# q and k fetched one head further ahead, W1 in eight smaller pieces, and the hash bits of both column halves in one bank

## The chip, the core and the metric

The kernel runs on one core of one Trainium2 chip. The time is that of the device, in microseconds, for one launch. Most executions of one kernel agree closely, but three runs of this one spread over 13 us (below). A tensor product is made by TensorE (PE), element work by VectorE (DVE), ScalarE (ACT) and GpSimd (POOL); transfers are issued from the queues of SyncE (SP) and POOL and are carried by the same 16 DMA engines.

## What is computed

```python
def _attn_ref(q, k, v, proj):                      # 2 x 8 heads, 768 rows, head_dim 64
    scale = 1.0 / np.sqrt(D)
    q_bits = (np.einsum('bhsd,dk->bhsk', q, proj) > 0)      # 6 bits per row
    k_bits = (np.einsum('bhsd,dk->bhsk', k, proj) > 0)
    mask = q_bucket[:, :, :, None] == k_bucket[:, :, None, :]
    scores = scale * np.matmul(q, k.transpose(0, 1, 3, 2))
    scores = np.where(mask, scores, -1000000000.0)
    attn = softmax(scores)
    return np.matmul(attn, v)

x = attention output as (2, 768, 512)
x = u + relu(norm(u) @ w_ch1) @ w_ch2,  u = x + real(fft2(x))
out = u2 + relu(u2 @ w_ch),  u2 = x + w_tok_r @ (x cos(x w_theta)) + w_tok_i @ (x sin(x w_theta))
```

All of it is float32. The kernel gets that precision by splitting each operand into a high part and the rest, and multiplying three times.

## The kernel before

The program runs through four stages: attention over 16 heads (to about 270 us of the span), the two Fourier products and the norm (to about 345 us), the network with W1 and W2, and the token mixing. The change touches attention and the transfer of W1 that runs beside it.

**The slots.** `schedule()` lays attention out in slots. A slot is one tile of 128 query rows; a head has six, t = 0 to 5. In a slot PE makes the tile's scores (four products, lines 771 and 772), then the six transposes (746) of the tile two slots back in two units "eta" and "etb", then four products with v (786, 787) for the tile five slots back, which add up in one bank `OT`, and last the slot's extra units. There are two kinds of these: "bits" of the next head in slots 0 and 1 (three products each, lines 724 to 726, one column half each), and "back" in slots 3 and 5 (three transposes, line 757). The units share three PSUM banks in turn (`ring`), and a unit waits until the one three before it has been copied out.

**What follows on the other engines.** For each tile DVE takes the row maxima of the scores (`negmax`, 993), makes from them the factor and bias of the exponential (`affine`, 996, a 128x2 operation whose inputs both lie in SBUF), and subtracts the high part of the transposed tile (`ETL`, 1003, twice). ACT copies out the transposed tile (`ETH`, 619), then takes the exponential (`E`, 626), which needs `affine`, and in slots 1 and 4 it then copies out the finished bank of the v products (`OS`, 635). PE can start the next v products, in slots 2 and 5, only when that copy is done. DVE also makes `einv` (1022, 1024) once a head, in slot 3.

**The mask.** The bits of q and k of the next head enter its scores as 12 further rows of the second product (`QM`, `KM`). ACT copies the bits from PSUM to `MB` (643), one half in slot 0 and one in slot 1. POOL turns them into rows (`mask_rows`, 507: `MR`, 24x768), and SP moves these rows under q and k with two transfers (426, 427). The first head's rows are made by DVE (1017).

**POOL, per head, in order:** `finish` (516, 519) of the head before, `mask_rows` for head h + 1, `scale_q` (492) for head h + 2, the split of q and k of head h + 2 into high and low part (`split_top`: 500 and 502, the latter with two inputs in SBUF), `finish`, `split_v` (535, 537). POOL takes these as soon as what they wait for is there; nothing ties them to a slot. In slots 2 and 5 it also issues one of the waiting transfers in `early`: twelve tables, then W1 in four transfers of 1 MB, so that two go out per head.

**SP, per head, in order:** `move_away(h)` (410, 411), `load_qk(h + 1)` (392), `move_in(h)` (417, 418), `move_mask(h)` (426, 427), `load_v(h + 1)` (397). It waits in order: a transfer that waits holds all behind it. `QK` has two buffers, filled by turns.

## Time and profile before

| what | value |
|---|---|
| runs, us | 796.34, 809.35, 806.29 |
| median, us | 806.29 |
| the profiled execution, us | 805.94 |
| its span, us | 803.8 |
| mean granted clock of PE, share of full speed | 0.968 |
| busy share of the span: PE, DVE, ACT, POOL | 93%, 55%, 40%, 36% |
| POOL mask rows (L507), 15 of them, mean ns | 2933 |
| idle of POOL before them, waiting for ACT's copy of the bits, us | 43.6 |
| idle of PE before the scores, waiting for the mask transfer (3 times), us | 9.1 |
| idle of PE before the v products, waiting for ACT's OS (13 times), us | 4.0 |

The profile is of one execution; its times are counted from the start of its span. A row of the trace gives the start, the duration, the engine, the line and what is written from what; a bracket at its end says how long the engine had been idle and what released it. Matmuls overlap in the records, so PE's pace is read from the distance between starts.

### The profile page before, as it was taken

The page shows a single profiled execution, that of the slowest core. Times are in us where ns is not written, and L with a number is a line of the kernel's source. Part 1 is how long each engine was busy: PE and PEld are TensorE (multiplying, and loading weights), DVE is VectorE, ACT ScalarE, POOL GpSimd, SP SyncE. Part 2 cuts the span into 40 slices and gives each one's busy share as a digit, 9 for nine tenths or more (in the row PEclk, how much of TensorE's full clock was granted, in tenths as well). Part 3 has the DMA queues.
Part 4 walks back from the last instruction along what each step waited for, and adds up shares of the span by engine and source line. Part 5 has one row for each costly group of instructions (what it writes and reads, how often), then busy time and mean ns, then how long its engine had stood idle before and what let it go on. Part 6 is the DMA issues. An engine that isn't in the chain of part 4 may idle for free.

```text
span 803.8 us, 10972 instructions
## 1 busy us (share of the span) xinstructions
PE 745.3 (93%) x3826; PEld 625.6 (78%) x3826; DVE 445.5 (55%) x770; ACT 318.3 (40%) x659; POOL 286.9 (36%) x275
## 2 busy tenths in 40 slices
PE   4999989989999769799999999999995998999998
PEld 2788888878898557688888888888874787888876
DVE  2998997889998688522212122211127565855433
ACT  2889887879899211211111111011014342322201
POOL 3788977668772376335000000200002114312100
PEclk9999999999999869799999999999998999999999
DMA  5366548733430134712000001300002231000002
GB/s 146 94 154 170 136 93 203 192 89 87 113 73 5 53 114 135 210 40 78 1 1 1 0 1 47 99 0 1 1 31 81 60 92 40 1 14 21 19 27 78
DMA packets 44679, 56.25 MB, mean 70 GB/s; under 512 B 15956, under 2 KB 27860, under 8 KB 44116
## 3 DMA queue, kind: packets, MB, share of 16 engines
q1 hardware_dynamic: 38100, 41.65, 19.3%
q0 software_dynamic: 6528, 13.92, 6.1%
q8 instruction: 32, 0.52, 0.3%
q14 instruction: 19, 0.16, 0.1%
HBM read 38.65 MB, written 3.15 MB: 52 GB/s over the span
## 4 chain that ended last, share of the span: by engine, by line
PE 75%; DVE 14%; issue 4%; DMA 3%; ACT 2%; POOL 1%; SPq 1%; ACTq 0%; POOLq 0%
PE PS L724 20%; PE PS L726 19%; PE PS L725 19%; DVE negmax L993 4%; PE PS L746 3%; DVE ETL L1003 3%; PE PS L786 3%; PE PS L771 2%; PE PS L772 2%; PE PS L787 2%; DVE affine L996 2%; DMA KM<-MR 2%; PE PS L907 1%; PE PS L914 1%; PE PS L757 1%
## 5 line engine op out<-in xcount | busy, mean ns | idle before, releaser
L1113 DVE SCALAR_TENSOR_TENSOR HL<-PS,HH 128x512 fp32r<-128x512 f32 x48 | 33.2, 692 | 188.6 <-ACT HH L687 188.6
L687 ACT ACTIVATE HH<-PS 128x512 fp32r<-128x512 f32 x48 | 28.7, 598 | 210.4 <-PE PS L726 210.4
L626 ACT ACTIVATE E<-PS,affine 128x768 f32<-128x768 f32 x96 | 95.3, 992 | 35.7 <-DVE affine L996 33.0
L993 DVE TENSOR_REDUCE negmax<-PS 128x1 f32<-128x768 f32 x96 | 90.9, 947 | 28.4 <-PE PS L772 27.5
L1003 DVE TENSOR_TENSOR ETL<-PS,ETH 128x384 fp32r<-128x384 f32 x192 | 97.1, 545 | 1.2 <-ACT ETH L619 1.2
L619 ACT ACTIVATE ETH<-PS 128x384 fp32r<-128x384 f32 x192 | 83.4, 488 | 9.6 <-PE PS L746 9.0
L746 PE MATMUL PS<-ident,E 128*128 128x128 f32 x576 | 82.1, 276 | 4.2 <-DVE ETL L1003 4.2
L771 PE MATMUL PS<-TOPH,TOPL 128*128 128x512 f32 x192 | 69.8, 364 | 9.4 <-DMA KM<-MR 9.1
L724 PE MATMUL PS<-UTH,W1H 128*128 128x512 f32 x192 | 76.8, 400 | 1.7 <-DVE UTL L1096 1.7
L786 PE MATMUL PS<-ETH,VHL 128*128 128x384 f32 x192 | 73.2, 381 | 4.9 <-ACT OS L635 4.0
L725 PE MATMUL PS<-UTL,W1H 128*128 128x512 f32 x192 | 75.9, 396 | 0.0
L726 PE MATMUL PS<-UTH,W1L 128*128 128x512 f32 x192 | 75.8, 395 | 0.0
L726 PE MATMUL PS<-W2H,HL 128*128 128x512 f32 x192 | 74.7, 389 | 0.0
L724 PE MATMUL PS<-W2H,HH 128*128 128x512 f32 x192 | 74.7, 389 | 0.0
L725 PE MATMUL PS<-W2L,HH 128*128 128x512 f32 x192 | 74.7, 389 | 0.0
L746 PEld LDWEIGHTS PS<-ident,E 128*128 128x128 f32 x576 | 65.9, 141 | 7.6 <-DVE ETL L1003 7.1
L587 POOL TENSOR_TENSOR ZF<-X,SC 128x512 f32<-128x512 f32 x24 | 30.5, 1291 | 107.2 <-ACT SC L708 107.2
L787 PE MATMUL PS<-ETL,VHL 128*128 128x384 f32 x192 | 65.2, 340 | 0.0
L772 PE MATMUL PS<-KM,QM 76*128 76x512 f32 x192 | 63.3, 349 | 0.0
L724 PE MATMUL PS<-ZH,WTH 128*128 128x512 f32 x144 | 59.9, 416 | 0.0
L507 POOL TENSOR_SCALAR MR<-MB,gamma 24x768 fp32r<-24x768 f32 x15 | 44.0, 2933 | 43.6 <-ACT MB L643 43.6
L726 PE MATMUL PS<-ZH,WTL 128*128 128x512 f32 x144 | 57.0, 396 | 0.0
(167 smaller groups left out, 1530.2 us busy)
## 6 DMA issues: line engine op xcount, KB each, us to landing
stage<-in_moe_w_ch_dram SPq DMA_DIRECT2D x36, 256.0 KB, 2.6
QK<-in_qk_dram SPq DMA_DIRECT2D x16, 384.0 KB, 4.0
W1H<-in_moe_w_ch_dram POOLq DMA_DIRECT2D x4, 1024.0 KB, 10.4
W2H<-in_moe_w_ch_dram POOLq DMA_DIRECT2D x4, 1024.0 KB, 8.8
QM<-TOPH SPq DMA_DIRECT2D x16, 192.0 KB, 3.0
KM<-TOPL SPq DMA_DIRECT2D x16, 192.0 KB, 3.6
VR<-in_v_dram SPq DMA_DIRECT2D x16, 192.0 KB, 2.8
TOPL<-QM SPq DMA_DIRECT2D x16, 192.0 KB, 2.7
```

Of the source, the lines that this page charges most:

```text
L619: nc.scalar.activation(ETH[:, t // HALF, k * HALF:(k + 1) * HALF, (t % HALF) * P:(t % HALF + 1) * P], bank, ACT.Copy).then_inc(s_eth, 1)
L626: nc.scalar.activation(E[:, tile % NE, :], s_bank(tile)[:, 0:S], ACT.Exp, bias=affine[:, t, 1:2], scale=affine[:, t, 0:1], accum_out=esum[ ...
L724: nc.tensor.matmul(dst, hl, hr, start=start, stop=False)
L725: nc.tensor.matmul(dst, hl, lr, start=False, stop=False)
L726: return nc.tensor.matmul(dst, ll, hr, start=False, stop=stop)
L746: last = nc.tensor.transpose(bank[:, j * P:(j + 1) * P], E[:, tile % NE, (first + j) * P:(first + j + 1) * P], ident[:])
L771: nc.tensor.matmul(dst, TOPL[:, h % 3, c], TOPH[:, h % 3, lo:hi], start=True, stop=False)
L772: last = nc.tensor.matmul(dst, QM[:, h % 2, c], KM[:, h % 2, lo:hi], start=False, stop=True)
L786: nc.tensor.matmul(OT, VHL[:, h % 2, j, :], ETH[:, c, j, :], start=(j == 0), stop=False)
L787: last = nc.tensor.matmul(OT, VHL[:, h % 2, j, :], ETL[:, c, j, :], start=False, stop=(j == QT - 1))
L993: nc.vector.tensor_reduce(negmax[:, t, 1:2], s_bank(tile)[:, 0:S], AX_X, ALU.max, negate=True).then_inc(s_max, 1)
L1003: nc.vector.tensor_tensor(ETL[where], blocks(ring(unit_no[kind, h, t])[:, 0:HC]), ETH[where].bitcast(F32), ALU.subtract).then_inc(emptied[ ...
```

## The change

Five edits, of which some only follow from others.

1. Bits. Both column halves of a head's bits are made in slot 0, into one bank: the first half's into rows 32 to 55, the second's into rows 0 to 23, by products 56 columns wide that have zeros beside the 24 that count. There are six products as before. ACT copies 56x384 once, and POOL's mask rows are 56x384 in place of 24x768. `gamma`, `proj2` and `sign` are widened to fit.
2. The mask rows are moved by four transfers of 12x384 in place of two of 12x768.
3. SP loads q and k of head h + 2 where it loaded those of head h + 1, and those of head 2 at the start. The buffers and the waits are the same.
4. W1 comes in eight transfers of 0.5 MB.
5. `early` gets a turn in slot 2 only up to head 7. The twelve tables go out in heads 0 to 5 as before, four pieces of W1 in heads 6 and 7, and four in slot 5 of heads 8 to 11.

```diff
-    slots = [(None, None, None, [("bits", 0, i) for i in range(2)])]
+    slots = [(None, None, None, [("bits", 0, 0)])]
...
-        if h + 1 < NH and t < 2:
-            units.append(("bits", h + 1, t))
+        if h + 1 < NH and t == 0:
+            units.append(("bits", h + 1, 0))
...
-            "w1": [(W1H[:, c, :], w1[c * P:(c + 1) * P, :]) for c in range(DT)],
+            "w1": [(W1H[:, c, i * FF // 2:(i + 1) * FF // 2], w1[c * P:(c + 1) * P, i * FF // 2:(i + 1) * FF // 2])
+                   for c in range(DT) for i in range(2)],
...
-                sp.wait_ge(s_ring, done["bits", h, 1])
+                sp.wait_ge(s_ring, done["bits", h, 0])
...
-                sp.dma_start(QM[D:D + NM, b].bitcast(F32), MR[0:NM].bitcast(F32)).then_inc(s_mask, 16)
-                sp.dma_start(KM[D:D + NM, b].bitcast(F32), MR[NM:2 * NM].bitcast(F32)).then_inc(s_mask, 16)
+                for i in range(2):
+                    c, r = slice(i * HC, (i + 1) * HC), (1 - i) * 32
+                    sp.dma_start(QM[D:D + NM, b, c].bitcast(F32), MR[r:r + NM].bitcast(F32)).then_inc(s_mask, 16)
+                    sp.dma_start(KM[D:D + NM, b, c].bitcast(F32), MR[r + NM:r + 2 * NM].bitcast(F32)).then_inc(s_mask, 16)
...
             move_mask(0)
+            load_qk(2)
             load_v(1)
...
-                if h + 1 < NH:
-                    load_qk(h + 1)
+                if h + 2 < NH:
+                    load_qk(h + 2)
...
-                pool.wait_ge(emptied["bits"], 2 * (h + 1))
-                pool.wait_ge(s_mask, 32 * h)
+                pool.wait_ge(emptied["bits"], h + 1)
+                pool.wait_ge(s_mask, 64 * h)
...
-                if slot and t in (2, 5) and early:
+                if slot and (t == 5 or t == 2 and h < 8) and early:
...
-                        nc.scalar.activation(MB[:, c], ring(unit_no[u])[0:2 * NM, 0:HC], ACT.Copy).then_inc(emptied["bits"], 1)
+                        nc.scalar.activation(MB[:], ring(unit_no[u])[0:MP, 0:HC], ACT.Copy).then_inc(emptied["bits"], 1)
...
-                    last = product(bank[0:2 * NM, 0:HC], projH[:], TOPH[:, h % 3, c], projL[:], TOPL[:, h % 3, c], True, True)
+                    r = h % 3
+                    product(bank[0:MP, 0:HC], projH[:, 0:MP], TOPH[:, r, 0:HC], projL[:, 0:MP], TOPL[:, r, 0:HC], True, False)
+                    last = product(bank[0:MP, 0:HC], projH[:, 32:PROJ], TOPH[:, r, HC:S], projL[:, 32:PROJ], TOPL[:, r, HC:S], False, True)
```

How the instructions stand on PE at the end of slot 0 of head 2, before: the last two v products, the three bits products of one half, and the scores of slot 1.

```order
L786 MATMUL PS<-ETH,VHL 128x384
L787 MATMUL PS<-ETL,VHL 128x384
L724 MATMUL PS<-TOPH,projH 24x384 [waits s_top,s_ol]
L725 MATMUL PS<-TOPL,projH 24x384
L726 MATMUL PS<-TOPH,projL 24x384
L771 MATMUL PS<-TOPH,TOPL 128x512 [waits s_mask,s_exp,s_in,s_away]
L772 MATMUL PS<-KM,QM 128x512
```

The same place in the changed kernel (its line numbers are six higher):

```order
L792 MATMUL PS<-ETH,VHL 128x384
L793 MATMUL PS<-ETL,VHL 128x384
L730 MATMUL PS<-TOPH,projH 56x384 [waits s_top,s_ol]
L731 MATMUL PS<-TOPL,projH 56x384
L732 MATMUL PS<-TOPH,projL 56x384
L730 MATMUL PS<-TOPH,projH 56x384
L731 MATMUL PS<-TOPL,projH 56x384
L732 MATMUL PS<-TOPH,projL 56x384
L777 MATMUL PS<-TOPH,TOPL 128x512 [waits s_mask,s_exp,s_in,s_away]
L778 MATMUL PS<-KM,QM 128x512
```

All six products now stand in slot 0; in slot 1 the scores of slot 2 follow directly on the v products.

On POOL, before, from head 6's mask rows to its second transfer of W1:

```order
L507 TENSOR_SCALAR MR<-MB,gamma 24x768
L492 TENSOR_SCALAR QK<-QK 64x768
L500 CAST TOPH<-QK 128x768
L502 TENSOR_TENSOR TOPL<-QK,TOPH 128x768
L561 DMA W1H<-in_moe_w_ch_dram 128x2048
L516 TENSOR_TENSOR OS_68<-OL_67 128x192
L519 TENSOR_TENSOR X<-OS_68,einv 128x3x64
L535 CAST VHL<-VR 128x6x64
L537 TENSOR_TENSOR VHL<-VR,VHL 128x6x64
L561 DMA W1H<-in_moe_w_ch_dram 128x2048
```

After, the same stretch has the same order, with the first row half as long and the pieces of W1 half as wide:

```order
L514 TENSOR_SCALAR MR<-MB,gamma 56x384
L499 TENSOR_SCALAR QK<-QK 64x768
L507 CAST TOPH<-QK 128x768
L509 TENSOR_TENSOR TOPL<-QK,TOPH 128x768
L568 DMA W1H<-in_moe_w_ch_dram 128x1024
```

On SP, before, from the second head's mask to its next load of q and k:

```order
L426 DMA QM<-MR 12x768 [waits s_mr]
L427 DMA KM<-MR 12x768
L397 DMA VR<-in_v_dram 128x6x64 [waits s_vs]
L410 DMA QM<-TOPH 64x768 [waits s_s,s_top]
L411 DMA KM<-TOPL 64x768
L392 DMA QK<-in_qk_dram 128x768 [waits s_top]
```

After; the last row now brings q and k of the head behind the one that it brought before:

```order
L432 DMA QM<-MR 12x384 [waits s_mr]
L433 DMA KM<-MR 12x384
L432 DMA QM<-MR 12x384
L433 DMA KM<-MR 12x384
L401 DMA VR<-in_v_dram 128x6x64 [waits s_vs]
L414 DMA QM<-TOPH 64x768 [waits s_s,s_top]
L415 DMA KM<-TOPL 64x768
L396 DMA QK<-in_qk_dram 128x768 [waits s_top]
```

Nothing else moved on SP but the one load of `QK` for head 2 at the start.

## Rows read from the trace of the kernel before

**Rows 1.** Busy time by stretch: engine columns, granted clock, DMA share, GB/s
```profile
60.00:90.00 30.00, 29.52 (x198) 26.80 (x197) 27.66 (x55) 27.44 (x62) 26.22 (x26) 1.00 0.58 139
120.00:150.00 30.00, 28.29 (x179) 25.56 (x177) 24.20 (x48) 24.65 (x56) 19.29 (x20) 0.94 0.93 231
```

**Rows 2.** Timeline of PE, one head from slot 2 on: start us, us, engine
```profile
63.07 0.40 PE L771 MATMUL PS<-TOPH,TOPL 128*128 128x512 f32 x1
...
65.15 0.39 PE L771 MATMUL PS<-TOPH,TOPL 128*128 128x512 f32 x1
...
71.38 0.41 PE L786 MATMUL PS<-ETH,VHL 128*128 128x384 f32 x1 [0.25 <-ACT OS L635]
...
72.41 0.49 PE L771 MATMUL PS<-TOPH,TOPL 128*128 128x512 f32 x1
...
74.56 0.34 PE L724 MATMUL PS<-TOPH,projH 128*24 128x384 f32 x1
...
75.08 0.39 PE L771 MATMUL PS<-TOPH,TOPL 128*128 128x512 f32 x1
...
77.67 0.40 PE L771 MATMUL PS<-TOPH,TOPL 128*128 128x512 f32 x1
...
78.97 0.42 PE L786 MATMUL PS<-ETH,VHL 128*128 128x384 f32 x1
```

**Rows 3.** Timeline of ACT in the same head
```profile
70.76 0.48 ACT L635 ACTIVATE OS<-PS 128x384 f32<-128x384 f32 x1
...
78.18 0.48 ACT L635 ACTIVATE OS<-PS 128x384 f32<-128x384 f32 x1
78.55 0.46 ACT L643 ACTIVATE MB<-PS 24x384 f32<-24x384 f32 x1
```

**Rows 4.** Timeline of DVE: affine of slots 2, 3 and 5
```profile
64.98 0.51 DVE L996 SCALAR_TENSOR_TENSOR affine<-negmax 128x2 f32<-128x2 f32 x1
...
67.32 0.16 DVE L996 SCALAR_TENSOR_TENSOR affine<-negmax 128x2 f32<-128x2 f32 x1
...
71.57 0.82 DVE L996 SCALAR_TENSOR_TENSOR affine<-negmax 128x2 f32<-128x2 f32 x1
```

**Rows 5.** Timeline of POOL: mask rows of three heads, q's scaling, two splits
```profile
64.50 2.94 POOL L507 TENSOR_SCALAR MR<-MB,gamma 24x768 fp32r<-24x768 f32 x1 [1.43 <-ACT MB L643]
67.43 2.13 POOL L492 TENSOR_SCALAR QK<-QK 64x768 f32<-64x768 f32 x1
...
70.53 1.85 POOL L502 TENSOR_TENSOR TOPL<-QK,TOPH 128x768 fp32r<-128x768 f32 x1
...
74.69 1.03 POOL L537 TENSOR_TENSOR VHL<-VR,VHL 128x384 fp32r<-128x384 f32 x1
...
79.12 2.94 POOL L507 TENSOR_SCALAR MR<-MB,gamma 24x768 fp32r<-24x768 f32 x1 [1.41 <-ACT MB L643]
...
193.61 2.93 POOL L507 TENSOR_SCALAR MR<-MB,gamma 24x768 fp32r<-24x768 f32 x1 [2.91 <-ACT MB L643]
```

**Rows 6.** Timeline of POOL: mask rows of the next two heads
```profile
93.91 2.93 POOL L507 TENSOR_SCALAR MR<-MB,gamma 24x768 fp32r<-24x768 f32 x1 [1.41 <-ACT MB L643]
...
111.15 2.93 POOL L507 TENSOR_SCALAR MR<-MB,gamma 24x768 fp32r<-24x768 f32 x1 [4.32 <-ACT MB L643]
```

**Rows 7.** Timeline of DVE between these two: affine of slot 4
```profile
100.08 1.69 DVE L996 SCALAR_TENSOR_TENSOR affine<-negmax 128x2 f32<-128x2 f32 x1
```

**Rows 8.** Line 411, its 16 KM<-TOPL transfers: time to landing
```profile
DMA to landing us min/median/max: 3.0/3.6/9.1
```

**Rows 9.** Tile QK, its 16 transfers: time to landing
```profile
DMA to landing us min/median/max: 3.0/4.0/12.5
```

**Rows 10.** Timeline of PE: the longer of two waits during W1's transfers
```profile
135.52 0.76 PE L771 MATMUL PS<-TOPH,TOPL 128*128 128x512 f32 x1 [1.59 <-DMA KM<-MR]
```

**Rows 11.** Timeline of SP: the first head's last mask transfer
```profile
11.71 0.74 SPq L427 DMA_DIRECT2D KM<-MR  x1
```

**Rows 12.** Timeline of PE: the first scores
```profile
14.11 0.76 PE L771 MATMUL PS<-TOPH,TOPL 128*128 128x512 f32 x1 [6.15 <-DMA KM<-MR]
```

More of the change, by code:

```diff
@@ L24 @@
 NM = 2 * BITS
+MP = 56
+PROJ = 88
 SCALE = D ** -0.5
@@ L91, in program @@
     einv = put("einv", [P, NSTAT])
-    sign = put("sign", [P, 2 * NM])
-    proj2 = put("proj2", [P, 2 * NM])
-    projH = put("projH", [P, 2 * NM], F32R)
-    projL = put("projL", [P, 2 * NM], F32R)
-    gamma = put("gamma", [2 * NM, 2])
+    projH = put("projH", [P, PROJ], F32R)
+    projL = put("projL", [P, PROJ], F32R)
+    gamma = put("gamma", [MP, 2])
     stats = put("stats", [P, NT, 6])
@@ L108, in program @@
     OS = put("OS", [P, 2, HC])
+    sign = put("sign", [P, PROJ], F32, tail)
+    proj2 = put("proj2", [P, PROJ])
+    used[0] = tail + 4 * 2 * HC
     un_at = used[0]
@@ L111, in program @@
     region = used[0]
-    MB = put("MB", [2 * NM, S], F32, un_at)
+    MB = put("MB", [MP, HC], F32, un_at)
     nat = put("nat", [P, 2, QT, P], F32, tail)
@@ L138, in program @@
     KM = put("KM", [D + NM, 2, S], F32R)
-    MR = put("MR", [2 * NM, S], F32R)
+    MR = put("MR", [MP, HC], F32R)
     VR = put("VR", [P, 2, QT, D])
@@ L424, in move_mask @@
                 else:
-                    sp.wait_ge(emptied["bits"], 2)
-                sp.dma_start(QM[D:D + NM, b].bitcast(F32), MR[0:NM].bitcast(F32)).then_inc(s_mask, 16)
-                sp.dma_start(KM[D:D + NM, b].bitcast(F32), MR[NM:2 * NM].bitcast(F32)).then_inc(s_mask, 16)
+                    sp.wait_ge(emptied["bits"], 1)
+                for i in range(2):
+                    c, r = slice(i * HC, (i + 1) * HC), (1 - i) * 32
+                    sp.dma_start(QM[D:D + NM, b, c].bitcast(F32), MR[r:r + NM].bitcast(F32)).then_inc(s_mask, 16)
+                    sp.dma_start(KM[D:D + NM, b, c].bitcast(F32), MR[r + NM:r + 2 * NM].bitcast(F32)).then_inc(s_mask, 16)
             load_qk(0)
@@ L747, in unit @@
                 elif kind == "bits":
-                    c = slice(i * HC, (i + 1) * HC)
                     pe.wait_ge(s_top, 2 * (h + 1))
-                    if h == 0 and i == 0:
+                    if h == 0:
                         pe.wait_ge(s_proj, 3)
-                    last = product(bank[0:2 * NM, 0:HC], projH[:], TOPH[:, h % 3, c], projL[:], TOPL[:, h % 3, c], True, True)
+                    r = h % 3
+                    product(bank[0:MP, 0:HC], projH[:, 0:MP], TOPH[:, r, 0:HC], projL[:, 0:MP], TOPL[:, r, 0:HC], True, False)
+                    last = product(bank[0:MP, 0:HC], projH[:, 32:PROJ], TOPH[:, r, HC:S], projL[:, 32:PROJ], TOPL[:, r, HC:S], False, True)
                 elif kind == "back":
@@ L764, in _ @@
                     pe.wait_ge(s_in, 32 * (h + 1))
-                    pe.wait_ge(s_mask, 32 * (h + 1))
+                    pe.wait_ge(s_mask, 64 * (h + 1))
                     if tile >= 2:
@@ L1012, in _ @@
                     kind, h, i = u
-                    bank = ring(unit_no[u])
-                    c = slice(i * HC, (i + 1) * HC)
                     if kind == "bits" and h == 0:
                         dve.wait_ge(s_ring, done[u])
-                        nc.vector.tensor_scalar(MR[:, c], bank[0:2 * NM, 0:HC], gamma[:, 0:1], gamma[:, 1:2], ALU.is_gt,
+                        nc.vector.tensor_scalar(MR[:], ring(unit_no[u])[0:MP, 0:HC], gamma[:, 0:1], gamma[:, 1:2], ALU.is_gt,
                                                 ALU.mult).then_inc(emptied["bits"], 1)
@@ L1189, in constants @@
     half = np.arange(1, LH)
+    gamma = np.array([[0, 1]] * BITS + [[-TINY, 1]] * BITS + [[-TINY, -PEN]] * BITS + [[0, -PEN]] * BITS, dtype=np.float32)
     return {
         "ident": np.eye(P, dtype=np.float32),
-        "gamma": np.array([[0, 1]] * BITS + [[-TINY, 1]] * BITS + [[-TINY, -PEN]] * BITS + [[0, -PEN]] * BITS, dtype=np.float32),
-        "sign": np.tile(np.repeat(np.array([[1, -1, -1, 1]], dtype=np.float32), BITS, axis=1), (P, 1)),
+        "gamma": np.concatenate([gamma, np.zeros((32 - 2 * NM, 2), np.float32), gamma]),
+        "sign": np.tile(np.concatenate([np.zeros(32), np.repeat([1, -1, -1, 1], BITS), np.zeros(32)]).astype(np.float32), (P, 1)),
         "cs": parts(wave(np.cos, np.arange(S // 2), np.arange(KC), S)),
@@ L1221 @@
     rows = [_np.swapaxes(a, 2, 3) for a in (inputs["q"][:, :, order], inputs["k"])]
-    blocks = _np.zeros((P, 2 * NM), dtype=inputs["proj"].dtype)
-    blocks[0:D, 0:NM] = _np.tile(inputs["proj"], (1, 2))
-    blocks[D:P, NM:2 * NM] = _np.tile(inputs["proj"], (1, 2))
+    blocks = _np.zeros((P, PROJ), dtype=inputs["proj"].dtype)
+    blocks[0:D, 32:32 + NM] = _np.tile(inputs["proj"], (1, 2))
+    blocks[D:P, 32 + NM:32 + 2 * NM] = _np.tile(inputs["proj"], (1, 2))
     laid = dict(inputs, qk=_np.concatenate(rows, axis=2).reshape(NH, P, S), projb=blocks, moe2_w_tok_r=inputs["moe2_w_tok_r"][order][:, order],
```

1 line of the change is left out of this document (removed).

## The prediction
> **What bounds the kernel now.** I read the busy times by stretch first, because the change lies in attention alone. In a quiet stretch PE is busy for 29.5 of 30 us at full clock, DVE for 27.7. In the stretch in which W1 comes, the transfer engines are 93% busy, PE loses 1.7 us in 30, and the mean clock is 0.94 [rows 1]. So there are two things to follow: a quiet head, and what the heads around W1 lose.
>
> For the quiet head I take PE's timeline and mark where each slot's scores start: slot 2 at 63.07, slot 3 at 65.15, slot 0 of the next head at 72.41, slot 1 at 75.08, slot 2 at 77.67 [rows 2]. That is 14.60 us a head; by the mask rows on POOL it is 14.62 (64.50 to 79.12) [rows 5]. PE loses under half a microsecond of it, at 71.38, where the v products of slot 5 wait for ACT's OS [rows 2]. Behind this wait stands DVE's chain: `affine` of slot 3 ends at 67.48 [rows 4], OS of slot 4 starts 3.28 later at 70.76 [rows 3], the v products 0.62 after that at 71.38, and the next head's slot 0 another 1.03 later [rows 2]. PE and this chain are nearly level, so what is added to either shows.
>
> What delays `affine`: alone it takes 0.16 us. In slot 5 it takes 0.82 and ends at 72.39, just behind POOL's operation 502 (70.53 + 1.85 = 72.38) [rows 4, 5]. In slot 2 it ends at 65.49, 0.99 after POOL began the mask rows, which go on to 67.44 [rows 4, 5]. So 502, with two inputs, holds it to its end; the mask rows, with one, only for their first third. In slot 5 the hold is harmless, since PE then has the bits of slots 0 and 1 to do. In the head of 94 to 111 us it isn't: `affine` of slot 4 takes 1.69, 1.53 too much, and that head lasts 17.24 us, 2.6 more than a quiet one [rows 6, 7].
>
> **The transfers: what is gained.** From the mask rows at 79.12 to those at 193.61 are seven heads in 114.49 us; at 14.62 they would take 102.3 [rows 5]. The excess is 12.2 us. Part of it comes from the transfers: a KM<-TOPL takes up to 9.1 us to land (median 3.6), a QK up to 12.5 (median 4.0) [rows 8, 9], and PE waits for the mask behind them [rows 10]. With the halved pieces 1 MB goes out beside a head in place of 2, and q and k get a whole head more (14.6 us), above the worst 12.5. The rest are holds like that of rows 6 and 7, which come when POOL and DVE slip against each other. I take all 12.2 as gone and count the holds of the new alignment in full below. The other bound: only the 2.6 of rows 6 go, and 9.6 stay.
>
> **The start: what is lost.** The first head's last mask transfer is issued at 11.71 for 0.74 us, and PE starts at 14.11 [rows 11, 12]. Two more transfers now stand ahead of it. Transfers of half the size aren't in the trace; each costs between nothing more and 0.74, so 0 to 1.5 together. I take 1.5, as that is the nearest row. In later heads SP has time, since the mask rows come earlier. Loading q and k of head 2 there adds one issue behind them, with 14 us to spare.
>
> **The quiet head after the change**, from the start of slot 0 at time 0.
>
> *Slots 0 and 1.* Three products that took 0.52 (74.56 to 75.08) move in from slot 1, so slot 1 starts at 2.67 + 0.53 = 3.20 [rows 2]. PE's work per head stays the same.
>
> *Slot 2.* OS of slot 1 starts 3.10 after that slot's scores (75.08 to 78.18) [rows 2, 3], at 6.30; the v products of slot 2 can start 0.62 later, at 6.92. PE would be there 3.89 - 0.52 = 3.37 after slot 1 (75.08 to 78.97, less the three products) [rows 2], at 6.57. It loses 0.35 where it lost nothing: the bits in slot 1 were the cover. Slot 3 follows 0.78 behind these v products (2.08 from 63.07 to 65.15, less 1.30 from 77.67 to 78.97) [rows 2], at 7.70.
>
> *POOL.* The last of the six bits products starts at 2.15 + 5 x 0.175 = 3.02 and is through 0.34 later [rows 2]. ACT's one copy starts at 3.4, the mask rows 0.57 behind it (78.55 to 79.12) [rows 3, 5], at 3.97. Their duration is the one operation that the trace doesn't show. Bounds: half of 2.94 is 1.47, and 2.94 if nothing scales. POOL's split takes 1.85 for 768 columns and 1.03 for 384 [rows 5], a fixed part of 0.2; with this, (2.94 - 0.2) / 2 + 0.2 = 1.57, which I take. q's scaling follows at once, as q and k are there, and 502 starts 3.10 after it (67.43 to 70.53) [rows 5]: from 8.64 to 10.49.
>
> *Slot 3.* `affine` wants to start 1.91 after the scores (63.07 to 64.98) [rows 2, 4], at 9.61, in the middle of 502. It is held to 10.52, for 0.91. This is the collision that was harmless in slot 5; now it stands at the head of DVE's chain. OS of slot 4 follows at 13.80, the v products at 14.42, the next slot 0 at 15.45.
>
> A head takes 15.45 in place of 14.62. POOL does this split beside heads 0 to 13; head 0 starts up and I leave it as it is, so 13 x 0.83 = 10.8 us. ACT's saved copy and POOL's shorter mask rows are off this path and gain nothing; the shorter rows only bring 502 forward. W1's last pieces land later but still inside attention, and what reads them starts behind it: nothing.
>
> **The sum.** -12.2 + 1.5 + 10.8 = +0.1. The profiled execution took 805.94, 0.35 less than the median of 806.29, so I predict 806.
>
> **Rivals.**
> *The collision does no harm.* If 502 begins after 9.61, 1.0 later than I put it, `affine` of slot 3 ends at 9.77 and the next slot 0 stands at 9.77 + 3.28 + 0.62 + 1.03 = 14.70. The 13 heads then cost 1.0: 805.94 - 12.2 + 1.5 + 1.0 = 796.2. For it: 1.0 is little, and the mask rows may not shrink (2.94 would do it). Against: POOL's chain and PE's both hang on slot 0's bits, so they don't drift apart.
> *Slower: 502 comes later, but not late enough.* Up to a start of 9.61, each 0.1 us of delay holds `affine` 0.1 longer, in 13 heads. Just before that point the period is 16.4 and the time 806.0 + 12.6 = 818.6. It needs mask rows of 1.7 to 2.5 us or a late copy of ACT. For it: POOL's time for this shape is unknown between 1.47 and 2.94. Against: its other widths scale.
> *W1 still crowds.* 9.6 us stay: 815.6. For it: the tables' larger pieces were 0.6 MB, also two to a head, and I can't see a loss of more than 0.3 there, which speaks against.
>
> **A rule weighed.** The mask rows hold `affine` of slot 2 for 0.99 of their 2.94 us [rows 4, 5]. The Trainium skill (SBUF — State Buffer, "SBUF: two separate sides") says that the pair of ports shared by VectorE and GpSimd stays locked for the whole instruction. By the rows, slot 1's `affine` (wanted at 5.11) clears mask rows that began at 3.97. By the rule it would be held to their end, 5.54: 0.43 more on the way to slot 3 in 13 heads, 5.6 us, which would lift the first rival to 801.8 and leave the forecast alone, because there slot 3 is held to 10.52 in any case. The rows decide for me.
>
> **Chances.** Forecast 0.50, with a range of its own of 803 to 809 (mask rows 1.47 to 1.8, start 0 to 1.5). Collision harmless 0.27; later 502 0.15; W1 crowds 0.05; another way 0.03. The range of 794 to 815 reaches over the first rival with a cheap start and over most of the second. 2% is 790.2 and 822.4, about what a measurement of this kernel can tell from no change; none of the cases gets there alone: faster 0.04, same 0.92, slower 0.04.
>
> **What the changed profile would show.** If I am right: heads of 15.4 us evenly through attention; `affine` of slot 3 at about 1 us, ending with POOL's 502 (509 there); PE waiting for OS in slots 2 and 5; mask rows of 1.6 us; no wait of POOL for q and k and no landing of 9 us; first scores at 15.6. Heads of 14.7 with a short `affine` in slot 3 mean the first rival, heads over 15.6 with mask rows over 1.7 the second, uneven heads from 100 to 180 us the third. I am wrong altogether if the six bits products take more than 1.05 us, or if heads change length after W1 has landed.

## The result, and the profile after

| | kernel before | changed kernel |
|---|---|---|
| runs, us | 796.34, 798.75, 806.29, 809.35 | 807.44, 811.91, 812.04, 815.81 |
| median, us | 802.52 | 811.97 |
| the profiled execution, us (its span) | 805.94 (803.8) | 815.81 (813.3) |
| start of the last head's three back transposes, us of the span ("end of attention" below) | 270.55 | 270.50 |
| first transpose of normalized rows, us | 315.33 | 322.30 |

The ratio is 1.0152, with an interval of 1.0104 to 1.0199, which is 12 us. Within 2%, but slower, where I had forecast no change at all. Measured again on another chip, the changed kernel took 814.33 us and the kernel before 807.39, with a ratio of 1.0148 (e9, below). The two kernels' distance is 7 to 9 us by the medians of all runs and 12 us by the ratios. The ratios use fast runs alone, those within about 1.5% of a kernel's fastest; the kernel before scatters so widely that this takes off its slow end, so I give both readings where they differ.

In attention nearly every mark that I had named stands in the trace. One head on PE, from slot 0 to the next slot 0 (columns as in [rows 2]):

```profile
59.63 0.48 PE L777 MATMUL PS<-TOPH,TOPL 128*128 128x512 f32 x1
...
62.83 0.40 PE L777 MATMUL PS<-TOPH,TOPL 128*128 128x512 f32 x1
...
64.90 0.39 PE L777 MATMUL PS<-TOPH,TOPL 128*128 128x512 f32 x1
...
65.61 0.82 PE L752 MATMUL PS<-ident,E 128*128 128x128 f32 x6
66.53 0.41 PE L792 MATMUL PS<-ETH,VHL 128*128 128x384 f32 x1
...
67.31 0.39 PE L777 MATMUL PS<-TOPH,TOPL 128*128 128x512 f32 x1
...
74.15 0.41 PE L792 MATMUL PS<-ETH,VHL 128*128 128x384 f32 x1 [0.29 <-ACT OS L642]
...
75.18 0.48 PE L777 MATMUL PS<-TOPH,TOPL 128*128 128x512 f32 x1
```

From 59.63 the slots follow at 3.20, 5.27 and 7.68, and the next head at 15.55; I had 3.20, slot 3 at 7.70 and 15.45. In slot 2 the v products start 0.92 after the transposes, where they started 0.58 after them before (63.78 and 64.36 in that trace): that is the small stall of 0.35, though no bracket marks it. POOL in this head, and after it the last mask rows:

```profile
63.63 1.66 POOL L514 TENSOR_SCALAR MR<-MB,gamma 56x384 fp32r<-56x384 f32 x1 [1.78 <-ACT MB L649]
...
68.38 1.85 POOL L509 TENSOR_TENSOR TOPL<-QK,TOPH 128x768 fp32r<-128x768 f32 x1
...
79.17 1.65 POOL L514 TENSOR_SCALAR MR<-MB,gamma 56x384 fp32r<-56x384 f32 x1 [1.79 <-ACT MB L649]
...
234.47 1.66 POOL L514 TENSOR_SCALAR MR<-MB,gamma 56x384 fp32r<-56x384 f32 x1 [1.78 <-ACT MB L649]
```

DVE beside it (slot 1, slot 3, then `einv`):

```profile
64.73 0.16 DVE L1002 SCALAR_TENSOR_TENSOR affine<-negmax 128x2 f32<-128x2 f32 x1
...
68.22 0.96 DVE L999 TENSOR_REDUCE negmax<-PS 128x1 f32<-128x768 f32 x1 [0.33 <-PE PS L778]
69.21 1.03 DVE L1002 SCALAR_TENSOR_TENSOR affine<-negmax 128x2 f32<-128x2 f32 x1
...
71.09 0.16 DVE L1026 TENSOR_SCALAR einv<-esum 128x6 f32<-128x6 f32 x1
```

`affine` of slot 3 is held for 1.03 us and ends at 70.24, just behind POOL's 509 (68.38 + 1.85 = 70.23). Where [rows 4] had 0.82 in slot 5, the subtraction is long done. The mask rows take 1.66 (1.57 forecast). The stretches that answer to [rows 1]:

```profile
60.00:90.00 30.00, 28.84 (x187) 25.60 (x186) 25.66 (x50) 25.29 (x58) 22.20 (x23) 1.00 0.53 139
120.00:150.00 30.00, 28.85 (x188) 25.65 (x186) 25.66 (x51) 25.34 (x58) 20.82 (x22) 1.00 0.53 151
```

Both stretches are alike: in a quiet head PE is busy for less of the time (28.8 of 30 us, 29.5 before), and W1 disturbs nothing any more. KM<-TOPL now lands in 4.6 us at most (9.1 in [rows 8]), QK in 7.7 (12.5 in [rows 9]). From 63.63 to 234.47 are eleven heads in 170.84 us, 15.53 each.

So the profiled execution reached the end of attention exactly when the profiled execution of before did. And yet the kernel is 7 to 12 us slower. That was the question for the experiments.

### The profile page after: what moved, and what is told of

Its sections match the earlier page's. It is cut to its first block, busy times and chain, and to the rows that moved or that the text cites. A ratio compares the mean times of both kernels' runs of the same rounds, so it can differ in the third digit from the quotient of the medians.

```text
span 813.3 us, 10963 instructions
## 1 busy us (share of the span) xinstructions
PE 755.6 (93%) x3826; PEld 632.1 (78%) x3826; DVE 435.9 (54%) x769; ACT 315.2 (39%) x644; POOL 270.9 (33%) x279
## 3 DMA queue, kind: packets, MB, share of 16 engines
q1 hardware_dynamic: 38902, 41.72, 18.1%
## 4 chain that ended last, share of the span: by engine, by line
PE 80%; DVE 12%; issue 3%; ACT 2%; DMA 1%; SPq 1%; POOL 0%; ACTq 0%; POOLq 0%
PE PS L730 20%; PE PS L732 19%; PE PS L731 19%; PE PS L752 4%; PE PS L792 4%; DVE negmax L999 3%; PE PS L777 3%; PE PS L778 3%; PE PS L793 3%; DVE affine L1002 2%; DVE ETL L1009 2%; PE PS L913 1%; PE PS L920 1%; PE PS L763 1%; PE PS L804 1%
## 5 line engine op out<-in xcount | busy, mean ns | idle before, releaser
L731 PE MATMUL PS<-ZL,WTH 128*128 128x512 f32 x144 | 57.2, 397 | 0.0
```

The source lines that it names most:

```text
L731: nc.tensor.matmul(dst, hl, lr, start=False, stop=False)
```

## The experiments

"End" is the end of attention in the profiled execution of a kernel; "head 0" is the distance of the first two mask rows.

| kernel | median, us (runs, range) | end | head 0 | other heads |
|---|---|---|---|---|
| e1 before, unchanged | 804.39 (12, 797.39 to 812.72) | 270.79 | 14.27 | 14.6 to 18.77 |
| e2 bits alone | 811.36 (12, 809.78 to 822.67) | 271.92 | 12.54 | 15.53, once 15.92 |
| e3 transfers alone | 796.45 (6, 792.71 to 804.79) | 260.57 | 14.25 | 14.6 to 14.94 |
| e4 late split | 800.82 (12, 797.23 to 807.84) | 264.26 | 15.02 | 14.68 to 14.92 |
| e5 before, attention only | 282.40 (6, 278.26 to 286.35) | 263.05 | 14.23 | 14.6, once 17.23, once 15.60 |
| e6 changed, attention only | 287.39 (4, 287.30 to 288.81) | 271.53 | 12.49 | 15.54 |
| e7 transfers alone, attention only | 274.99 (5, 274.31 to 275.27) | 259.84 | 14.25 | 14.6 to 14.96 |
| e8 bits alone, attention only | 289.54 (4, 287.76 to 290.43) | 274.64 | 14.67 | 15.54, once 16.32 |
| e9 changed, again | 814.33 (6, 808.54 to 817.10) | 274.11 | 15.40 | 15.54 |
| e10 changed, attention only, small shift | 293.84 (6, 293.41 to 293.95) | 278.17 | 12.97 | 16.02 |
| e11 changed, attention only, large shift | 302.62 (6, 301.03 to 305.82) | 285.27 | 14.13 | 16.17 to 16.52, last 18.1 |
| e12 q and k ahead alone, attention only | 275.71 (6, 275.49 to 276.57) | 260.32 | 14.26 | 14.6 to 14.97 |
| e13 before, to the Fourier part | 340.02 (6, 335.07 to 344.68) | 263.59 | 14.26 | 14.6, once 17.23, once 16.17 |
| e14 changed, to the Fourier part | 346.60 (6, 341.79 to 347.61) | 273.47 | 14.72 | 15.54 |
| e15 transfers alone, to the Fourier part | 330.86 (5, 330.24 to 332.88) | 259.11 | 14.28 | 14.6 to 14.94 |
| e16 bits alone, to the Fourier part | 346.27 (6, 341.27 to 352.13) | 272.49 | 12.55 | 15.54, 16.47, 15.78 |

The kernel before took 803.63 us beside e1 to e4 (29 runs, 794.85 to 813.01), 803.58 beside e5 to e8, 807.39 beside e9 to e12 and 801.34 beside e13 to e16 (11 runs each); each of these four groups ran on one chip, and each group on another. The median of the kernel before moves by up to 6 us between chips, so small differences between groups are not resolved. A ratio below is to the kernel before on the same chip.

### The change taken apart: e1 to e4

e1 is the kernel before, unedited. e2 has edits 1 and 2 (bits and mask), e3 edits 3 to 5 (q and k ahead, W1 in eight pieces). e4 is the changed kernel with POOL's subtraction for TOPL moved behind the first `finish` of the head:

```diff
                 nc.gpsimd.tensor_copy(TOPH[:, r], QK[:, b]).then_inc(s_top, 1)
+                if h < 2:
+                    split_low_top(h)
+
+            def split_low_top(h):
+                b, r = h % 2, h % 3
                 pool.wait_ge(s_top, 2 * h + 1)
                 nc.gpsimd.tensor_tensor(TOPL[:, r], QK[:, b], ...
...
                 if slot and t == 3 and h:
                     finish(h - 1, 0)
+                if slot and t == 3 and h + 2 < NH:
+                    split_low_top(h + 2)
```

> The kernel before, unchanged, once more. In its first profile seven heads between 79 and 194 us lost 12.2 us against the quiet 14.62 each. Theory A (the prediction's): this loss is there in every execution; the heads from 79 to 194 take about 114 us again and the times lie near 806. Theory B: the first profile was one of its slower executions; the loss varies from run to run between about 2 and 12 us, and the times spread over 796 to 809. The stretch from the last attention product (270.5) to the first transposes of the normalised rows (315.3) took 44.8 us there; B expects it to vary too, with the granted clock.

Measured 804.39, a ratio of 1.0009 (0.9972 to 1.0047). The uneven heads of [rows 5, 6] come again in the profiled execution: 17.23, 18.77, 17.63 and 15.61 among heads of 14.6. That spoke for theory A, the spread of the times (797.39 to 812.72) for theory B: it decided nothing.

> Edits 1 and 2 alone: bits of both halves in slot 0, one copy, half-length mask rows, four mask transfers; q, k and W1 are fetched as before. If the collision with POOL's split in slot 3 is the cost: heads of 15.5 us throughout, as in the changed kernel, plus what W1's transfers add at 120 to 180 us (0 to 5, as the mask rows are now earlier and have 3 us more slack). Time against the kernel before: +5 to +14 us. If W1 or the earlier load is what makes the change slow, this kernel is level with the one before.

Measured 1.0114 (1.0082 to 1.0145), 7.7 us more than the 803.63 beside it (9 by the ratio), within the 5 to 14 expected.

> Edits 3 to 5 alone: q and k one head further ahead, W1 in eight pieces; bits and mask rows as before. If the bits edit carries the whole cost: heads of 14.6 us, without the uneven ones between 94 and 194 us, so that attention ends 9 to 12 us before the 270.5 of the first profile, and the time is 795 to 799. Rival: the uneven heads come from holds of affine by POOL that have nothing to do with transfers; then at least half of the 12 us stays, and the time is 799 to 806.

Measured 0.9874 (0.9829 to 0.9919), 7.2 us less (10 by the ratio). This version beats both kernels. Its heads are even (14.6 to 14.94), and in its W1 stretch q's scaling follows the mask rows at once, with no wait for QK. The profiled execution took 804.79, 8.3 us above this median; five of the six runs lie at 792.71 to 796.67.

> The changed kernel with one thing moved: POOL's operation 502 (509 there), the low part of q and k, is issued after the first finish of the head in place of before it. It then begins when back's first half is copied out, some 13 us into the head, beside slot 5's affine instead of slot 3's. If the hold in slot 3 sets the head: affine of slot 3 takes 0.16 us, heads go from 15.55 to about 14.7, the time falls by 13 x 0.85 = 11 us against the changed kernel, to about 800. If the 15.55 come from the bits order on PE alone (the wait for OS in slot 2), nothing moves.

Measured 0.9987 (0.9952 to 1.0023), 800.82 us: 11 to 14 us less than the changed kernel on its two chips, with heads of 14.8. POOL and DVE of its trace, one head (POOL first):

```profile
69.22 0.82 POOL L507 CAST TOPH<-QK 128x768 fp32r<-128x768 f32 x1
...
73.88 1.84 POOL L514 TENSOR_TENSOR TOPL<-QK,TOPH 128x768 fp32r<-128x768 f32 x1
```

```profile
70.98 0.16 DVE L1009 SCALAR_TENSOR_TENSOR affine<-negmax 128x2 f32<-128x2 f32 x1
...
71.99 0.16 DVE L1033 TENSOR_SCALAR einv<-esum 128x6 f32<-128x6 f32 x1
```

The subtraction, later by nearly 4 us, now lies in a gap of DVE's small operations, and `affine` of slot 3 takes 0.16 again. The collision is the cause of most of the slower head: of the 0.9 us between 14.6 and 15.54 it made 0.7. The other 0.2, some 2.6 us in 13 heads, stays in e4 and has another cause, which no run takes apart.

### Attention only: e5 to e8

The full kernels scatter over 10 us and more. So attention was measured alone, in a kernel that stops behind it:

```diff
             sp.wait_ge(s_x, 2 * NH)
+            for n in range(NT):
+                sp.dma_start(out[n // QT, ...], X[:, n, :]).then_inc(s_out[n % 3], 16)
+            for i in range(3):
+                sp.wait_ge(s_out[i], 16 * len(range(i, NT, 3)))
+            return
...
             finish(NH - 1, 1)
-            pool.wait_ge(s_pv, 2 * NH)
-            split_low(n_w1)
+            pool.wait_ge(s_high["w1"], 16 * len(highs["w1"]))
+            pool.wait_ge(s_table, 16 * len(tables))
+            return
```

PE, ACT and DVE return behind the loop over the slots.

> The kernel before, ended behind attention: after the last head's sums X is written to the output and nothing of the Fourier part, the MLP and the mixture is computed, so the time is that of attention with the same W1 and table transfers in it, plus the writing. It asks where the 8 us lie by which the changed kernel is slower than the kernel before, although both profiled executions reached the end of attention at 270.5 us. Theory A: attention costs in every execution what it cost in the profiled ones, and the 8 us arise behind it, where the clock comes back late. Then this kernel's timed executions lie with its profiled one, at about 270.6 plus the writing of X (some 12 us): 283, and its twin of the changed kernel has the same time within 1 us. Theory B: the 12 us that heads 2 to 9 lose to the transfers of W1 are a feature of the profiled executions or of a few, and a usual execution loses 4 to 6: then the timed ones are 6 to 8 us below the profiled one, about 276.

> The changed kernel, ended behind attention in the same way. Both theories give a head of 15.55 us and an end of attention at 270.5, about 283 us in all, since its 15 intervals are alike to 0.05 us and nothing in it varies. Against its twin of the kernel before: theory A the same time within 1 us, theory B slower by 6 to 8 us.

> The kernel before with the transfers' part of the change alone (q and k one head further ahead, W1 in eight pieces), ended behind attention in the same way. Both theories put its end of attention at 260.6, 273 us in all. Against its twin of the kernel before: theory A faster by 10 us, theory B by 2 to 4.

> The kernel before with the bits' part of the change alone (products in one bank), ended behind attention in the same way. Its profiled execution reached the end of attention at 271.9, so 284 us in all; against its twin of the kernel before theory A gives 1 us more, theory B 7 to 9 us more.

The kernel before took 282.40 us with a range of 8.1, the changed one 287.39, the one with the transfers' edits 274.99 with a range of 1.0, the one with the bits' edits 289.54. Theory A falls: it had the two kernels level within 1 us, and they are 5.0 us apart by the medians, 7.1 by the ratios (0.3573 to 0.3485). Theory B has the better of it but not its numbers: it expected 276 for e5 and a gain of 2 to 4 us in e7, which came to 7.4 by the medians and 5.8 by the ratios. The profiled execution of e5 speaks for what the range consists of: it was the fastest of its runs and lost only 3.8 us against e7 (209.09 to 205.32 us from the first mask rows to the last). POOL in the W1 stretch of e5:

```profile
126.47 2.94 POOL L512 TENSOR_SCALAR MR<-MB,gamma 24x768 fp32r<-24x768 f32 x1 [1.98 <-ACT MB L649]
...
130.31 2.15 POOL L497 TENSOR_SCALAR QK<-QK 64x768 f32<-64x768 f32 x1 [0.90 <-DMA QK<-in_qk_dram]
...
141.24 2.93 POOL L512 TENSOR_SCALAR MR<-MB,gamma 24x768 fp32r<-24x768 f32 x1 [0.88 <-ACT MB L649]
146.04 2.14 POOL L497 TENSOR_SCALAR QK<-QK 64x768 f32<-64x768 f32 x1 [1.87 <-DMA QK<-in_qk_dram]
...
156.84 2.93 POOL L512 TENSOR_SCALAR MR<-MB,gamma 24x768 fp32r<-24x768 f32 x1 [2.02 <-ACT MB L649]
```

And the same stretch of the profiled execution on which I had based the sum:

```profile
126.10 2.95 POOL L507 TENSOR_SCALAR MR<-MB,gamma 24x768 fp32r<-24x768 f32 x1 [1.98 <-ACT MB L643]
131.95 2.13 POOL L492 TENSOR_SCALAR QK<-QK 64x768 f32<-64x768 f32 x1 [2.91 <-PE PS L772]
...
143.93 2.93 POOL L507 TENSOR_SCALAR MR<-MB,gamma 24x768 fp32r<-24x768 f32 x1 [1.98 <-ACT MB L643]
150.64 2.13 POOL L492 TENSOR_SCALAR QK<-QK 64x768 f32<-64x768 f32 x1 [3.78 <-DMA QK<-in_qk_dram]
...
160.26 2.93 POOL L507 TENSOR_SCALAR MR<-MB,gamma 24x768 fp32r<-24x768 f32 x1 [0.84 <-ACT MB L643]
...
179.00 2.93 POOL L507 TENSOR_SCALAR MR<-MB,gamma 24x768 fp32r<-24x768 f32 x1 [5.20 <-ACT MB L643]
```

There POOL waits 3.78 us for q and k, the heads last 17.83, 16.33 and 18.74, and all of attention loses 11.4 us against e7. In e5 the writing and what surrounds the span add 15.2 us to the end of attention (278.26 - 263.05). On this scale the profiled execution of before, with 270.55, is an execution of 285.8 us, near the top of e5's range of 278.26 to 286.35. The usual one, 282.40, loses 7.4 us to the transfers (282.40 - 274.99). What theory B had as 4 to 6 is 7.4, or 5.8 by the ratios.

### The changed kernel again, and the collision moved: e9 to e12

> The changed kernel as it is, beside the kernel before on one chip. Ended behind attention the changed kernel took 287.4 and the kernel before 282.4 us; what lies behind attention was worth 803.6 - 282.4 = 521.2 us in the kernel before, 521.4 with the transfers' edits alone and 521.9 with the bits' edits alone. Theory A, the parts add up and the rest has the same price in all of them: 287.4 + 521.5 = 808.9, a ratio of 1.0066. Theory B, the changed kernel loses some 3 us more behind attention, where its profiled execution had its clock back 13 us later: 812, a ratio of 1.010 or more.

Measured 814.33 to 807.39: 6.9 by the medians, a ratio of 1.0148 (1.0071 to 1.0226), 12 us. That is over the 5.0 or 7.1 of attention again, and above both theories' times; A's ratio of 1.0066 lies outside the interval. But its trace shows one thing that the first did not: head 0 lasts 15.40 in place of 12.54, and attention ends at 274.11 in place of 270.50. DVE and POOL in head 0 of e9, then of the first profiled execution of the changed kernel:

```profile
25.71 1.61 DVE L1002 SCALAR_TENSOR_TENSOR affine<-negmax 128x2 f32<-128x2 f32 x1
```

```profile
25.49 1.81 POOL L509 TENSOR_TENSOR TOPL<-QK,TOPH 128x768 fp32r<-128x768 f32 x1
```

```profile
24.38 0.28 DVE L1002 SCALAR_TENSOR_TENSOR affine<-negmax 128x2 f32<-128x2 f32 x1
```

```profile
24.73 1.84 POOL L509 TENSOR_TENSOR TOPL<-QK,TOPH 128x768 fp32r<-128x768 f32 x1
```

It is the same collision in the head that I had left out. In the short case `affine` ends 0.07 us before the subtraction starts; in the other it comes 0.22 behind its start and is held for 1.61. Head 0 is then 2.2 to 2.9 us longer (14.67 in e8, 14.72 in e14, 15.40 here, against 12.5 in the first trace, e2, e6 and e16).

Which case comes goes with PE's pace at the start of this head. The subtraction starts 9.21 to 9.25 us after the first scores in all seven traces that have the bits' edits and no shift; `affine` starts 8.80 to 9.01 after them in the four short ones and 9.34 to 9.46 in the three long ones. The difference shows already at slot 1 of this head, whose first product took 0.40 to 0.55 us in the short ones and 0.63 in the long ones (first the trace after, then e9):

```profile
18.82 0.45 PE L777 MATMUL PS<-TOPH,TOPL 128*128 128x512 f32 x1
```

```profile
19.59 0.63 PE L777 MATMUL PS<-TOPH,TOPL 128*128 128x512 f32 x1
```

Why PE is faster there in some executions stays open.

e10 and e11 shift the subtraction on purpose, with one filling operation ahead of it (`range(1)`) and with three (`range(3)`):

```diff
+        s_junk = sem("s_junk")
...
-            split = [0]
+            split, junk = [0], [0]
...
                 nc.gpsimd.tensor_copy(TOPH[:, r], QK[:, b]).then_inc(s_top, 1)
+                for _ in range(1):
+                    pool.memset(UN[:, 1, :], 0.0).then_inc(s_junk, 1)
+                    junk[0] += 1
+                    pool.wait_ge(s_junk, junk[0])
                 pool.wait_ge(s_top, 2 * h + 1)
```

> The changed kernel ended behind attention (287.4 us, a head of 15.55), with one filling operation on POOL, a memset of 128x512, between the cast and the subtraction that makes TOPL, so that this subtraction starts 0.5 to 0.8 us later. Theory collision: it starts at 68.9 to 69.2 of the head that had it at 68.38, still ahead of slot 3's affine row (69.21), and holds it to its own end, now later by the same 0.5 to 0.8: a head of 16.1 to 16.3, 13 heads long, 294 to 298 us. Where the shift reaches 0.83 it has passed the affine row and the time falls instead to about 278. Rival, the head is set by something that this subtraction does not hold up (PE's work, the mask's way): the shift costs nothing, 287.4, or its length lies in POOL's slack.

POOL and DVE of e10:

```profile
70.62 0.52 POOL L515 MEMSET UN<- 128x512 f32 x1
71.22 1.84 POOL L519 TENSOR_TENSOR TOPL<-QK,TOPH 128x768 fp32r<-128x768 f32 x1
```

```profile
71.58 1.51 DVE L1016 SCALAR_TENSOR_TENSOR affine<-negmax 128x2 f32<-128x2 f32 x1
```

`affine` takes 1.51, ending with the subtraction at 73.1; a head takes 16.02 for 15.55. The subtraction starts 5.23 us after the mask rows (4.75 without the memset), 0.48 later; the hold is 0.48 longer, the head 0.47 longer. 13 x 0.47 = 6.1, and the time is 293.84, 6.4 above that of e6, measured on another chip. Head and time lie just under the 16.1 to 16.3 and 294 to 298 expected, as the memset shifted the subtraction by 0.48 and not by 0.5 to 0.8. What happens to this one operation passes whole into the time.

> The same with three such memsets, so that the subtraction starts 1.5 to 2.3 us later, at 69.9 to 70.7, behind slot 3's affine row. Theory collision: although POOL does more and does it later, the affine row takes 0.2 to 0.5 us again, the head falls to 14.7 to 14.9 and the time to 277 to 279 us. Rival, POOL's work as such is what makes a head longer: 16.5 or more a head, over 297 us. In between: the later subtraction or POOL's work behind it now holds another operation of VectorE (the affine row of slot 4, wanted 2.9 us behind that of slot 3) or comes late with v, and takes a part of the gain back.

Measured 302.62, where collision had 277 to 279 us. POOL and DVE of e11:

```profile
88.30 1.68 POOL L515 MEMSET UN<- 128x512 f32 x3
90.06 1.87 POOL L519 TENSOR_TENSOR TOPL<-QK,TOPH 128x768 fp32r<-128x768 f32 x1
```

```profile
89.26 0.16 DVE L1016 SCALAR_TENSOR_TENSOR affine<-negmax 128x2 f32<-128x2 f32 x1
...
90.27 1.69 DVE L1040 TENSOR_SCALAR einv<-esum 128x6 f32<-128x6 f32 x1
...
92.10 0.92 DVE L1013 TENSOR_REDUCE negmax<-PS 128x1 f32<-128x768 f32 x1
```

```profile
100.05 1.65 POOL L524 TENSOR_SCALAR MR<-MB,gamma 56x384 fp32r<-56x384 f32 x1 [1.79 <-ACT MB L660]
```

`affine` is free, as forecast. But 1 us behind it DVE has its other small operation, `einv`, which I had not looked at: it is wanted at 90.27, 0.21 behind the subtraction's start, and held to its end at 91.96. It delays slot 4's maxima by 1.5 us. The time that came, over 297 us with heads of 16.2 to 16.5, is near what the expectation had given its rival, POOL's work as such. The trace speaks against that rival: POOL is still idle for 1.79 us ahead of the next mask rows, as in the changed kernel (1.78), so its work does not fill the head. And the holds give the number: 15.55, less the 0.87 by which `affine` had been held, and the 1.53 of `einv` on top, make 16.2. The expectation was wrong in its number, and what it named in between occurred: the subtraction had been moved from one collision into the next. e4 moved it past both.

> The kernel before ended behind attention (282.4 us) with one of the two edits of the transfers: q and k one head further ahead, W1 in four pieces of 1024 KB as before. Both edits together gave 275.0. If the time goes into q and k that land late (the POOL wait for QK of 1.87 us ahead of the 15.6 us head), this gives all of it: 275 to 276. If it goes into the mask's and the halves' small transfers behind a large piece (the waits of PE for KM), it gives little: 280 to 282, with single heads of 17 us left.

Measured 275.71, as expected: q and k one head ahead give nearly all of the gain (6.7 of the 7.4 us by the medians). The 0.7 left for W1's smaller and later pieces is a difference between two chips and not resolved. The loss began with q and k that landed late.

### Where the rest lies: e13 to e16

These stop behind the Fourier part, when X is updated and the first four normalized tiles are made (PE returns ahead of the products with W1, the other engines at the same place; POOL splits W1 as before).

> The kernel before, ended behind the Fourier part: the MLP and the mixture are not computed, X is written out once the Fourier sums and the first four normalized rows are there. Ended behind attention it took 282.4 us; its profiled executions needed 44.8 and 47.1 us from the end of attention to the first transpose of normalized rows, so 330 to 335 us are expected here. Theory A: the Fourier part has the same price in all four kernels but for scatter, then what remains of the changed kernel's loss is scatter of whole runs. Theory B: it costs the changed kernel 2 to 4 us more.

> The changed kernel, ended behind the Fourier part in the same way (287.4 us when ended behind attention; 51.8 and 50.0 us from there to the first transpose of normalized rows in its profiled executions). Against its twin of the kernel before: theory A 5 us slower (4 to 6), theory B 7 to 9 us.

> The kernel before with the transfers' edits alone, ended behind the Fourier part. Behind attention it stood 7.4 us below the kernel before and in the whole 7.2 us: both theories expect 7 to 8 us less than the twin of the kernel before here.

> The kernel before with the bits' edits alone, ended behind the Fourier part. Behind attention it stood 7.1 us above the kernel before and in the whole 7.8 us: both theories expect 7 to 8 us more here.

The changed kernel is 6.6 us slower than its twin of before by the medians, between the two theories, and 8.3 by the ratios (0.4294 to 0.4190), within theory B's 7 to 9. The other expectations missed: e13 took 340.02 for 330 to 335; e15 is 9.2 us below it and e16 6.3 above it, for 7 to 8 each. In e14 attention had the long head 0 (14.72). Five of its six runs lie at 344.77 to 347.61 and one at 341.79. That the longer runs of e14 and e9 are those with the long head 0 is inferred from the profiled ones; the timed ones show no heads.

From the end of attention to the first transpose of normalized rows these four profiled executions need 46.8, 46.6, 46.6 and 46.5 us. That looks like one price of the Fourier part for all kernels, but it is not what whole kernels pay. POOL and DVE of e14, then POOL of the changed kernel:

```profile
315.72 1.26 POOL L543 TENSOR_TENSOR W1L<-stage,W1H 128x512 fp32r<-128x512 f32 x1 [1.03 <-DMA stage<-in_moe_w_ch_dram]
317.07 0.23 POOL L590 TENSOR_SCALAR rstd<-moments 128x1 f32<-128x1 f32 x1
```

```profile
317.99 0.55 DVE L1056 TENSOR_SCALAR UN<-X,moments,rstd 128x512 f32<-128x512 f32 x1 [3.88 <-POOL rstd L592]
```

```profile
313.16 0.23 POOL L580 TENSOR_SCALAR rstd<-moments 128x1 f32<-128x1 f32 x1 [2.41 <-DVE moments L1036]
```

In e13 to e16 the norm (`rstd`) starts right behind POOL's last split of W1, 43.5 to 43.8 us after the end of attention, although the moments of the first rows were ready at 34.4 to 39.0. In the seven profiles of whole kernels POOL is through with W1 earlier, and in six of them the norm waits for the moments, which come at 40.0 to 42.6. So the shortened kernels all stop at POOL, and cannot tell what the Fourier part costs in a whole one. There the same stretch took 44.8, 47.1 and 47.3 us in the three profiles without edits 3 to 5 (before, e1, e2) and 51.8, 50.0, 51.6 and 49.6 in the four with them (changed kernel, e9, e3, e4).

What is known of the distance is then this. Attention gives 5.0 us by the medians and 7.1 by the ratios, and a long head 0 adds 2.2 to 2.9 where it comes. The whole kernels are 6.9 and 9.4 apart by the medians, which that covers, and 12 by both ratios, of which 2 to 5 us stay unexplained. That they lie in the stretch behind attention is likely from the seven profiles, but not shown: the timed runs of e3 are 7.2 us below the kernel before in whole and 7.4 in attention alone, so by the medians its edits cost nothing behind attention.

## Why the prediction was wrong

**The bits' part was right, to a few tenths.** Start and 13 heads were to cost 1.5 + 10.8 = 12.3 us. Measured, with the transfers' edits in both kernels: 287.39 - 274.99 = 12.4 (e6, e7). From the second mask rows to the last, 13 heads, e6 takes 202.07 us and e7 191.07: 11.0 for the 10.8. The hold was 1.03 for 0.91, and its cause was confirmed by e4 and e10. That the first scores came at 15.48 for 15.6 is partly luck: they scatter by over 1 us between profiles (14.01 to 15.36 in eight with two mask transfers, 15.48 to 16.60 in ten with four), and their means are 1.6 apart for the 1.5. That a head was to cost 0.83 and cost 0.9 holds for its size; e4 leaves 0.2 of it to something other than the hold.

**The step that failed is the first term, "I take all 12.2 as gone".** It was read from one execution, and it differs from execution to execution: 3.8 us in the profiled e5, 4.1 in e13, 10.4 in e1, 11.4 in the first profile, and 7.4 in the median of the timed runs (e5 against e7), or 5.8 by the ratios. The profiled execution's time was no warning, 0.35 us from the median that I had: its slow attention was partly made up for behind it, where it took 44.8 us to the normalized rows and e1 took 47.1. The spread of 13 us over three runs was the warning. The sum for attention with 7.4 is -7.4 + 12.3 = +4.9, against 5.0 measured; by the ratios it is -5.8 + 12.3 = +6.5, against 7.1. Between the two profiled executions of the first measurement the term came true, and both reached the end of attention at 270.5; for the usual execution of the kernel before it did not. And 811.97 lies in the wide range of 794 to 815 by luck, as that range was drawn to reach over two rivals that did not occur.

**A second, smaller step: "head 0 starts up and I leave it as it is".** Head 0 holds the same two operations, and there the change put them within 0.1 to 0.3 us of each other. By the mask rows it comes out at 12.5 or at 14.7 to 15.4. The long case adds 2.2 to 2.9 us.

**What stays open.** By the ratios the whole kernels are 12 us apart, and attention, with both steps in it, gives 7, or 10 with a long head 0. The forecast took the stages behind attention as unchanged ("W1's last pieces land later but still inside attention, and what reads them starts behind it: nothing"); whether this step holds, no run here shows.

**The rivals.** "The collision does no harm" was wrong about the phase: the mask rows did shrink. "502 comes later, but not late enough" was right as a mechanism, as e10 shows, and did not occur here except in head 0. What I gave as the point from which the first rival decides, 502 starting after `affine`, is only half of it: e11 shows that 502 must also clear `einv`. "W1 still crowds" was wrong; the heads are even. The case that occurred, W1 crowding less before than I had read, was not among my rivals; the bound of 2.6 us in the text stood for W1 still crowding after the change.

**The rule weighed.** `affine` of slot 1 (64.73, 0.16) runs in the middle of the mask rows (63.63 to 65.29) without a hold. The Trainium skill (SBUF — State Buffer, "SBUF: two separate sides") says that the loser of the shared ports blocks for the whole instruction. For POOL's one-input mask rows the trace disagrees; for its two-input subtraction, whose holds end with it in every row above, it agrees.

## What to carry to other kernels

A loss that is to be removed must be sized over many executions, not over the profiled one: cut the kernel behind the stage and time the stage alone, which here left 1.0 and 1.5 us of scatter in two of the four kernels and showed 6 to 7.4 where one profile had shown 12.2. And look at what sets the end of the shortened kernel: e13 to e16 ended on a wait that the whole kernel does not have. Where two engines are level, write down for each wide two-input POOL operation which small VectorE operations with all operands in SBUF will want to start while it runs, in the first head too, and past the first gap also; a shift of 0.5 us in 13 heads is 6 us either way. And take a change apart: here one half was worth -6 to -10 us and the other +7 to +12, and the half alone beats both kernels.

## What the runs showed of the hardware

What POOL's operation holds up is selective. Beside the two-input subtraction (1.85 us) VectorE's `affine` and `einv`, which read and write SBUF alone, wait to its end (1.03, 1.51, 1.61, 1.69 us for an operation of 0.16), whereas the maxima, which read PSUM, ran in their usual 0.96 us (68.22 in the trace after, with the subtraction from 68.38). Beside three memsets `affine` took 0.16 (89.26 in e11), beside the later part of the mask rows too. Two one-input operations held `affine` for a part of their time only: the mask rows of 24x768 for 0.99 of 2.94 us [rows 4, 5], q's scaling for 0.84 of 2.15 (head 0 of the changed kernel, where `affine` took 0.62 from 21.83 beside a scaling from 21.61).

A transfer of half the size did not cost half on SP's queue. Four mask transfers of 12x384 in the changed kernel's first head took 0.83, 0.74, 0.71 and 0.71 us:

```profile
10.98 0.83 SPq L432 DMA_DIRECT2D QM<-MR  x1
...
13.39 0.71 SPq L433 DMA_DIRECT2D KM<-MR  x1
```

The two of 12x768 had taken 0.83 and 0.74 (the latter [rows 11]), so the upper bound was the right one to take.

PE's clock comes back at different times behind the same pause. The stretches of the kernel before, then of the changed kernel (the columns of [rows 1]; the third number from the end is the granted clock):

```profile
295.00:305.00 10.00, 10.00 (x44) 7.45 (x44) 7.08 (x12) 1.16 (x3) 6.76 (x6) 0.61 0.34 120
305.00:315.00 10.00, 8.86 (x47) 6.70 (x46) 9.72 (x22) 2.46 (x5) 7.75 (x14) 1.00 0.34 106
```

```profile
295.00:305.00 10.00, 10.00 (x39) 7.54 (x39) 6.83 (x11) 0.77 (x2) 6.81 (x5) 0.50 0.35 124
305.00:315.00 10.00, 10.00 (x30) 7.98 (x29) 6.25 (x11) 0.88 (x2) 5.71 (x7) 0.50 0.33 102
```

After a pause of 4.88 us at the end of attention, the same in both, and one in the Fourier part (5.33 us before, 5.01 after), PE was at half speed (1.2 GHz) in the changed kernel through all of 295 to 315, in the kernel before only to somewhere in 295 to 305. From the end of attention to the normalized rows that made 51.8 us against 44.8. Whether the change has a part in it is not shown. Over the seven profiles of whole kernels the stretch took 44.8 to 47.3 us without edits 3 to 5 and 49.6 to 51.8 with them, but the profiled executions of e3 and e4 are 8.3 and 6.6 us above the medians of their kernels, so they may be uncommon ones. What decides when the clock returns in an execution stays open, and so does what makes q and k land late in some executions and not in others.
